# Soft-MoE attention kernel: keys and values of a batch pair loaded and pooled as 128 partitions of neighbouring groups, heads separated by transposes of 128 columns

## What is computed

```python
Sp = S // pool                                     # 576 // 8 = 72
k_p = k.reshape(B, H, Sp, pool, D).mean(axis=3)
v_p = v.reshape(B, H, Sp, pool, D).mean(axis=3)
scores = scale * np.matmul(q, k_p.transpose(0, 1, 3, 2))
scores = scores - np.max(scores, axis=-1, keepdims=True)
attn = np.exp(scores)
attn = attn / (np.sum(attn, axis=-1, keepdims=True) + 1e-09)
return np.matmul(attn, v_p).astype(np.float32)
```

## Time and profile before

| | us |
|---|---|
| median of 3 runs | 739.06 |
| lowest, highest | 737.74, 741.77 |
| span of the profiled execution | 738.6 |
| PE, DVE, ACT, POOL busy in it | 686.6, 465.3, 335.3, 138.6 |
| chain that ended last: PE, DVE, DMA | 75%, 14%, 4% |

### The profile page before, as it was taken

One profiled execution on the slowest core, in us unless ns is written; L12 is line 12 of the kernel. 1 busy time (PEld: TensorE's weight loads), 2 busy tenths in 40 slices (PEclk: granted clock), 3 DMA queues, 4 the chain that ended last, 5 costly groups with the idle time before them and its releaser, 6 DMA issues.

```text
span 738.6 us, 11129 instructions
## 1 busy us (share of the span) xinstructions
PE 686.6 (93%) x3931; PEld 552.3 (75%) x3931; DVE 465.3 (63%) x692; ACT 335.3 (45%) x580; POOL 138.6 (19%) x147
## 2 busy tenths in 40 slices
PE   4479999999999599789999999999999999999998
PEld 2468988888985243568888888888888888888886
DVE  5789897995756464976645545446464454644644
ACT  1236766767751224445434443443444344434442
POOL 1575775761221000920000000000000000000000
PEclk8569999999999879899999999999999999999999
DMA  7887879764667992000100101001010010100101
GB/s 202 209 210 210 219 217 223 189 230 207 234 223 283 429 425 116 1 0 1 58 0 1 58 0 58 0 0 57 0 57 0 0 57 0 50 8 0 58 1 57
DMA packets 31366, 80.28 MB, mean 109 GB/s; under 512 B 6496, under 2 KB 14688, under 8 KB 28512
## 3 DMA queue, kind: packets, MB, share of 16 engines
q1 hardware_dynamic: 31328, 79.76, 33.5%
HBM read 70.32 MB, written 9.44 MB: 108 GB/s over the span
## 4 chain that ended last, share of the span: by engine, by line
PE 75%; DVE 14%; DMA 4%; issue 4%; POOL 2%; ACT 1%; DVEq 0%; ACTq 0%
PE bank L1263 17%; PE bank L1265 17%; PE bank L1264 17%; PE bank L1129 5%; PE bank L1248 4%; DVE kp L761 4%; DMA kvbuf<-in_v_dram 3%; PE bank L1112 2%; PE bank L1199 2%; DVE ex L820 2%; PE bank L1093 2%; PE bank L1219 1%; DVE mx L808 1%; DVE cT L935 1%; PE bank L1039 1%
## 5 line engine op out<-in xcount | busy, mean ns | idle before, releaser
L1263 PE MATMUL bank<-w_hi,r_hi 128*128 128x512 f32 x576 | 227.3, 395 | 6.5 <-DVE r_lo L982 6.5
L1264 PE MATMUL bank<-w_lo,r_hi 128*128 128x512 f32 x576 | 226.0, 392 | 0.0
L1265 PE MATMUL bank<-w_hi,r_lo 128*128 128x512 f32 x576 | 225.9, 392 | 0.0
L979 DVE TENSOR_TENSOR win_sb<-win_sb 128x512 f32<-128x512 f32 x144 | 105.1, 730 | 175.0 <-ACT win_sb L736 173.9
L736 ACT ACTIVATE win_sb<-bank 128x512 f32<-128x512 f32 x144 | 86.1, 598 | 236.7 <-PE bank L1248 236.7
L1263 PEld LDWEIGHTS bank<-w_hi,r_hi 128*128 128x128 f32 x576 | 109.0, 189 | 32.2 <-DVE r_lo L982 9.3
L1265 PEld LDWEIGHTS bank<-w_hi,r_lo 128*128 128x128 f32 x576 | 109.3, 190 | 23.0
L1264 PEld LDWEIGHTS bank<-w_lo,r_hi 128*128 128x128 f32 x576 | 109.3, 190 | 23.0 <-issue 0.2
L982 DVE TENSOR_TENSOR r_lo<-win_sb,r_hi 128x512 fp32r<-128x512 f32 x144 | 104.2, 724 | 15.0
L745 ACT ACTIVATE r_hi<-win_sb 128x512 fp32r<-128x512 f32 x144 | 91.0, 632 | 13.1
L1129 PE MATMUL bank<-vx,aT 72*128 72x96 f32 (+1 forms) x640 | 70.6, 274 | 5.0 <-issue 4.3
(11 more groups left out here) (134 smaller groups left out, 583.3 us busy)
## 6 DMA issues: line engine op xcount, KB each, us to landing
late<-in_moe_w_dram SPq DMA_DIRECT2D x8, 2048.0 KB, 16.3
kvbuf<-in_k_dram SPq DMA_DIRECT2D x16, 576.0 KB
kvbuf<-in_v_dram SPq DMA_DIRECT2D x16, 576.0 KB
out_dram<-win_sb SPq DMA_DIRECT2D x36, 256.0 KB, 2.1
qbuf<-in_q_dram SPq DMA_DIRECT2D x8, 1024.0 KB, 10.9
early<-in_moe_w_dram SPq DMA_DIRECT2D x4, 2048.0 KB, 11.8
early_third<-in_moe_w_dram SPq DMA_DIRECT2D x2, 2048.0 KB, 11.7
win_sb<-in_moe_w_in_dram SPq DMA_DIRECT2D x4, 1024.0 KB, 5.8
```

The costliest lines, as they stand in the source:

```text
L979: dve.tensor_tensor(sq_sb[:, f % 2, :], r_sb[:, f % 2, :], r_sb[:, f % 2, :], ALU.mult).then_inc(sq_ready, 1)
L1263: pe.matmul(acc, r2_hi[:, f % 2, toks], w_hi[:, f, :], start=(f == 0), stop=False)
L1264: pe.matmul(acc, r2_hi[:, f % 2, toks], w_lo[:, f, :], start=False, stop=False)
L1265: last = pe.matmul(acc, r2_lo[:, f % 2, toks], w_hi[:, f, :], start=False, stop=(f == F2C - 1))
```

## The change

A load brings three neighbouring groups of keys for both batches and all heads: partition (batch, head, x) holds the groups 9x to 9x+8 of its head, and one third of them is a load of 128 partitions with 3 x 512 values (6 KB) in one run, 768 KB. There are 3 loads of keys and 3 of values for a pair. DVE sums them in one instruction a load and copies the result beside itself, so that a group has its 64 columns twice; POOL makes the last sum twice to the same end. Values go to a new buffer `vp`. PE transposes each group's 128 partitions x 128 columns; the two copies put the same columns on the lower and the upper 64 partitions, and ACT copies the even heads from the lower and the odd ones from the upper. Since values are now pooled with (batch, head, x) on the partitions, they are transposed a second time from `vT` to give `vx` (`values_natural`).

Keys of pair i are pooled in steps 9i-7, 9i-5 and 9i-3 and turned two steps later, together with values. In a step of PE the transposes of keys and values and the product with phi stand ahead of the product with values, and the turning of the attention weights comes behind it. `load_q(i, 1)` is issued behind four loads of the next pair.

```diff
-    KPP = PH // KCH
+    GH = P // PH
+    GL = KEYS // GH
+    PIECES = 3
...
+        kvbuf = sb("kvbuf", [P, RING, GP, ROW], where=att)
+        kp = sb("kp", [P, GL, 2, HD], where=att)
+        vp = sb("vp", [P, GL, 2, HD], where=att)
...
+        def key_step(i, u):
+            return TPP * i - 5 + 2 * u if i else 0
...
+        def value_step(i, u):
+            return TPP * i - 5 + 2 * u if i else (1, 1, 2)[u]
...
+        def pool_step(i, u):
+            return key_step(i, u) - 2
...
+        def natural_step(i):
+            return TPP * i if i else 3
...
+        def phi_step(i):
+            return TPP * i + 1 if i else 3
...
-        kv_v = [t.rearrange("b h (g r) d -> g b h (r d)", r=POOL) for t in (k, v)]
+        def kv_rows(which, i, u):
+            rows = (k, v)[which][2 * i:2 * i + 2].rearrange("b h (x g r) d -> (b h x) g (r d)", x=GH, r=POOL)
+            return rows[:, GP * u:GP * (u + 1), :]
...
-                sp.dma_start(kvbuf[:, c % RING], kv_v[which][:, bb, h0:h0 + KCH, :]).then_inc(kv_in[c % RING], 16)
+                        sp.wait_ge(k_pooled, 2 * (PIECES * i0 + u0) + 1)
+                sp.dma_start(kvbuf[:, c % RING], kv_rows(which, i, u)).then_inc(kv_in[c % RING], 16)
...
                         load_kv(1, i + 1, u)
+                load_q(i, 1)
...
-                pool.tensor_tensor(vx_of[i % 3][:, a, SLOTS:SLOTS + 2 * HD].rearrange("g (t d) -> g t d", t=2),
-                                   vb[:, :, 0:HD], vb[:, :, HD:2 * HD], ALU.add).then_inc(v_pooled, 1)
+                if i:
+
+                    pool.wait_ge(vT_ready, PIECES * i)
+                for copy in range(2):
+                    pool.tensor_tensor(vp[:, GP * u:GP * (u + 1), copy, :], vb[:, :, 0:HD], vb[:, :, HD:2 * HD],
+                                       ALU.add).then_inc(v_pooled, 1)
...
+                act.wait_ge(kT_ready, PIECES * i + u + 1)
+                for h in range(2):
+                    mine = k_bd[i % 2][HD * h:HD * (h + 1), :, KEYS * h:KEYS * (h + 1)]
+                    act.activation(keys_of(mine, u), turned_half(key_bank(i, u), h), ACT.Copy).then_inc(kT_kept, 1)
...
+                for h in range(2):
+                    act.activation(keys_of(vT[HD * h:HD * (h + 1)], u), turned_half(value_bank(i, u), h), ACT.Copy).then_inc(vT_kept, 1)
...
+                    act.activation(vx_of[i % 3][:, HP * half:HP * (half + 1), SLOTS:SLOTS + 2 * HD],
+                                   natural_bank(i, half)[0:KEYS, :].rearrange("g (a f) -> g a f", a=HP), ACT.Copy).then_inc(vn_kept, 1)
...
+                for i, u in pieces_with(key_step, n):
+                    keep_keys(i, u)
+                for i, u in pieces_with(value_step, n):
+                    keep_values(i, u)
+                for i in range(PAIRS):
+                    if n == natural_step(i):
+                        keep_natural(i)
...
-                dve.reduce_sum(kp[:, 2 * a:2 * a + 2, :],
-                               kvbuf[:, slot, heads].rearrange("g h (r d) -> g h d r", r=POOL), AX.X).then_inc(k_pooled, 1)
...
+                groups = kp[:, GP * u:GP * (u + 1)]
+                dve.reduce_sum(groups[:, :, 0, :], kv_groups(slot), AX.X).then_inc(k_pooled, 1)
+                dve.wait_ge(k_pooled, 2 * (PIECES * i + u) + 1)
+                dve.tensor_copy(groups[:, :, 1, :], groups[:, :, 0, :]).then_inc(k_pooled, 1)
...
+                for i in range(PAIRS):
+                    if n == phi_step(i):
+                        dve.wait_ge(vphi_ready, i + 1)
+                        dve.tensor_copy(head_logits(vx_of[i % 3][:, :, :].rearrange("g a f -> g (a f)"), PH // 2, 2 * VC, "a t s"),
+                                        phi_bank(i)[0:KEYS, :].rearrange("g (a t s) -> g a t s", t=2, s=SLOTS)).then_inc(vphi_kept, 1)
...
-                for i, a in pieces_at(n, False):
-                    pool_keys(i, a)
...
+                for i, u in pieces_with(pool_step, n, 1):
+                    pool_keys(i, u)
...
+            def turn_pooled(pooled, out, u):
+                for a in range(GP):
+                    twice = pooled[:, GP * u + a].rearrange("p c d -> p (c d)")
+                    last = pe.transpose(out[:, P * a:P * (a + 1)], twice, ident[:, :])
+                return last
...
+                pe.wait_ge(k_pooled, 2 * (PIECES * i + u + 1))
+                if i:
+                    pe.wait_ge(aT_kept, 2 * tiles_turned(key_step(i, u)))
+                turn_pooled(kp, key_bank(i, u), u).then_inc(kT_ready, 1)
...
+                        last = pe.transpose(natural_bank(i, half)[0:KEYS, P * a:P * (a + 1)], vT[:, HP * half + a, :], ident[:, :])
+                    last.then_inc(vn_ready, 1)
...
-                t = n - 3
-                if 0 <= t < TILES:
-                    pe.wait_ge(a_ready, t + 1)
...
-                    for g in range(2):
-                        if t:
-                            pe.wait_ge(aT_kept, 2 * (t - 1) + g + 1)
-                        for a in range(HB):
-                            last = pe.transpose(bank[A_B[g]][0:KEYS, P * a:P * (a + 1)], ex[:, t % 3, HB * g + a, :], ident[:, :])
-                        last.then_inc(aT_ready, 1)
+                for i, u in pieces_with(key_step, n):
+                    turn_keys(i, u)
+                for i, u in pieces_with(value_step, n):
+                    turn_values(i, u)
+                for i in range(PAIRS):
+                    if n == natural_step(i):
+                        values_natural(i)
+                    if n == phi_step(i):
+                        values_phi(i)
                 t = n - 4
                 if 0 <= t < TILES:
                     i = t // TPP
                     if t % TPP == 0:
+                        pe.wait_ge(vn_kept, 2 * (i + 1))
                         pe.wait_ge(vphi_kept, i + 1)
                     if t:
...
+                t = n - 3
+                if 0 <= t < TILES:
+                    pe.wait_ge(a_ready, t + 1)
...
+                        if t:
+                            pe.wait_ge(aT_kept, 2 * (t - 1) + g + 1)
+                        for a in range(HB):
+                            last = pe.transpose(bank[A_B[g]][0:KEYS, P * a:P * (a + 1)], ex[:, t % 3, HB * g + a, :], ident[:, :])
+                        last.then_inc(aT_ready, 1)
```

More of the change, by code:

```diff
@@ L371, in parts, with by_dve, values_pooled @@
+        def by_dve(i, u):
+            return i == 0 and u == 1
+        def values_pooled(i, u):
+            if by_dve(i, u):
+                return v_pooled_dve, 2
+            return v_pooled, 2 * sum(not by_dve(ii, b) for ii in range(i + 1) for b in range(PIECES if ii < i else u + 1))
         def parts(t):
@@ L575, in normalise @@
                 pool.tensor_tensor(e, e, r, ALU.mult).then_inc(a_ready, 1)
-            mine = [a for a in range(PIECES) if not by_dve(0, a)]
-            for step, a in enumerate(mine):
-                pool_values(0, a, step)
+            mine = [u for u in range(PIECES) if not by_dve(0, u)]
+            for step, u in enumerate(mine):
+                pool_values(0, u, step)
             for n in range(STEPS):
@@ L1018, in turn_values @@
[L1018 to L1028 removed]
+                return min(max(n - 3, 0), TILES)
```

215 lines of the change are left out of this document (87 added, 128 removed).

## The result

The changed kernel takes **752.55 us** (median of 4 runs, 751.75 to 757.15) where the kernel before took 739.97 in the same session (737.74 to 741.77): a ratio of 1.0175, 95% interval 1.0135 to 1.0215. It is slower, by less than 2% but clear of the noise, and the median lies above the forecast range of 731 to 747. The profiled span is 750.0 us against 738.6, so the two traces can be set against each other: 11.4 us are to be found.

The account below looks back on a forecast made before the run. Attention was taken as bound by loads at its start, then DVE, then PE, and the experts by weight loads; -11.9 + 2 x (3.0 + 0.4) + 3.1 + 1.9 = -0.1 us gave 739.0 us, range 731 to 747.

Parts of the forecast that it names:

- The experts' part: Stretch after attention, to 284 us: bound by weight loads, it passes on attention's shift whole and keeps its length, 0 us.
- Loads and start: Attention's start up to tile 10: loads of 128 partitions on all engines reach 400 GB/s, gaining 11.9 us.
- sub 10: Start of tile 10's subtraction of its row maxima, a mark of progress: forecast at 76.3 us instead of 88.16.
- The loads stay slow: Rival for the start: 16 engines used but only 240 GB/s, tile 10 at 81.9, total 744.5 us; chance 0.25 with similar waits.
- loads as before: Rival for the start: loads stay at 192 GB/s, start gains at most 2 us, 748 to 749 us; chance 0.07.
- PE's clock stays up: Rival for the start: no 1.2 GHz stretch, tile 10 at 72.3, total 735.0 us; chance 0.20.
- The pooling step: Loop steps pooling keys: product waits for logits, two steps take 10.33 us, six 32.2 instead of 29.2, 3.0 lost.
- the rival in which it does not bind: Rival for pooling steps: the product's wait for logits costs nothing, six take about 28.2, total 726 us; chance 0.05.
- The other three steps of a pair: Steps of a pair of batches outside the six with pooling: PE's changed transposes and a wait add 0.4 us a pair.
- The step without pooling: Steps from tile 28 to 35: copies and logits delay the product, 4.55 us against 4.05, 31.85 for seven, 3.1 lost.
- The tail: Tile 35's subtraction to the last product's end: 14.1 us where it took 12.2, 1.9 lost.
- sub 28: Start of tile 28's subtraction of its row maxima, a mark of progress; after it no keys are pooled.

Follow-up runs that it names:

- experiment 4: Changed kernel with TensorE's old order (weights turned before the product with values) only in the steps after the last tile's scores: 745.77 us, ratio 1.0071.
- experiment 7: Changed kernel with TensorE's old order throughout, plus unused identity products filling two gaps (step 4 and after the slot sums): 724.29 us, ratio 0.9783.
- experiment 3: Changed kernel plus unused identity products on TensorE before the product's wait: two in nearly all steps, 750.55 us; eight only at long gaps, 747.89 us.
- experiment 2: Changed kernel with ACT copying outputs ahead of turned weights, 748.33 us; then also DVE taking logits before pooling, 740.11 us.
- experiment 1: Changed kernel with the old order of TensorE's step and the copies that go with it; loads and pooling stay changed: 728.92 us, ratio 0.9819.
- the second part of experiment 2: Changed kernel with ACT copying outputs ahead of turned weights and DVE taking logits before pooling: 740.11 us, ratio 0.9971.

## Why the prediction was wrong

- **The experts' part and "nothing else in the later parts moves": wrong by 2.4 us.** It was taken as bound by loads, yet it moves with PE's clock: 1.65 us are the tail's half clock running on behind the last product, the rest is longer half clock at the experts' products. These gained 1.7 us in experiment 4 and 2.9 in experiment 7 once the clock before them was up.
- **Loads and start: right in size, for the wrong reason.** 400 GB/s was forecast and 383 measured; sub 10 came 13.9 us earlier instead of 11.9. The rise came from the partitions written, not from 16 engines, so that the size came out was luck. "The loads stay slow" and "loads as before" are out. Half of "PE's clock stays up" came true: at the start the clock stood at 1.00 until 20 us, and a single stretch of 3.4 us below it followed, where the kernel before stood at half clock from 14 to 41 us. Part of the 13.9 us is thus probably clock; it was not measured apart.
- **The pooling step: right in mechanism, and in size only at full clock.** 32.2 us for six were worked out; without half clock they take 32.84 (experiment 3), but in the changed kernel 35.4 and 34.0. The wait for the logits was there (2.40 us idle), and the rival in which it does not bind is out.
- **The other three steps of a pair: under-sized.** +0.4 was forecast, 18.25 - 16.97 = +1.3 measured. With the old order 0.7 of it stay: this is the added work. The other 0.6 go with the order.
- **The step without pooling: right.** 31.85 forecast, 32.32 measured, and experiment 2 shows that its cause is ACT's order.
- **The tail: mechanism right, size not.** 14.1 was forecast, 17.98 measured. ACT's copy of a group's slot sums stands between the copies of weights and outputs (PE waited 1.36 us for it); that was not in the prediction's chain. Then half clock: 2.83 + 2.08 + 1.57 us at 1.2 GHz for 1.54 + 1.16 + 1.04 at full clock, 2.7 us.
- **The step that failed** is that each wait was charged at its own length. The prediction kept the clock for the start and did not ask what new idle time does to it in a loop that had stood at 1.00 from 73 to 222 us. Six waits of 1.3 to 2.2 us, three of them followed by half clock, cost 3.75 us of clock in the two pairs; the tail's cost about 2.7, and 1.65 right behind it. That makes 8.1 of the 11.5 us by which the sum missed. Another 0.8 are half clock at the experts' products, which no run traces to these waits. The rest is 2 x 0.6 for the pooling steps and 2 x 0.85 for the others, 0.5 after sub 28 and 1.2 in the tail, less the 2.0 that the start gained beyond its forecast. What decides whether a wait is followed by half clock stays open.

Taken by its parts, the change was two: a layout that brings keys and values in faster, with sub 10 13.9 us earlier and 2.3 us more work in the two pairs, and an order on PE that the layout does not need, as experiment 1 shows, and that cost 21 us by the spans (750.0 against 729.0).

## What to carry to other kernels

When a change makes TensorE wait where it had been working without a gap, charge the wait and, as a risk beside it, the work behind it at half clock (here three of six such waits were followed by 3.4 us of it); look for the granted clock of each stretch, also of the stage after the one changed. Before an operation that waits for another engine's last result, put work that is ready; which of two blocks stands first can be worth more than what they do. Let a load write all 128 partitions, in each transfer: this, and not the length of its runs or the number of engines, set its rate here.

## What the runs showed of the hardware

- Eight products of no use in front of three waits of a pair raised the granted clock from 0.95 to 1.00 over 102 us. With two, 1.1 to 1.8 us of idle time remained, and so did half-clock stretches. The length of one wait does not tell whether the clock falls: after 1.16 us it fell in experiment 7 and after 1.17 in the same place of experiment 1 it did not, nor after 2.04 in the second part of experiment 2.
- Partitions written set the DMA rate: 2.7 to 3.1 GB/s each, with 72, 64 or 128 of them. With the 64 + 8 split all engines read busy (share 1.09) at the lowest rate of all (201 GB/s), so a DMA share near 1 tells nothing of whether the rate is what it could be.
- A small copy on DVE can wait for POOL. In experiment 1 the copy of pooled keys took 1.79 us once, 0.29 us while POOL is idle:

```profile
29.48 2.88 POOL L582 TENSOR_TENSOR kvbuf<-kvbuf 128x768 f32<-128x768 f32 x2 [1.69 <-DMA kvbuf<-in_v_dram]
...
29.65 1.79 DVE L789 COPY kp<-kp 128x192 f32<-128x192 f32 x1
```

POOL's row holds two additions, of which the first ends at 31.29; the copy ends at 31.44. In the changed kernel copies that start inside such an addition (of 1.81 us) end about 0.15 us after it too: 78.13 + 0.35 = 78.48 after 76.52 + 1.81 = 78.33. The Trainium skill (Trainium Architecture — The Big Picture, What this means for kernel authors) says that DVE and GpSimd share a pair of ports by an exclusive lock; the rows of the copies agree. DVE's poolings were not held back: the one at 86.93 takes 2.83 us beside POOL's additions, and 2.77 with POOL idle. The copy of experiment 1 lasted 1.5 us longer than one alone, and the subtraction behind it is the one for which PE then waited 2.3 us, with half clock after it.
